# First batch's heads in three rounds of query tiles, with three token chunks behind them, and w1 loaded without a ring

## The reference

```python
scores = (1 / np.sqrt(D)) * np.matmul(q, k.transpose(0, 1, 3, 2))
cum = np.cumsum(np.maximum(s, 0.0), axis=-1)
bias = -(cum[:, :, :, None] - cum[:, :, None, :])
scores = np.where(causal, -1e9, scores + np.minimum(bias, 0.0))
attn = softmax(scores)                     # with 1e-9 added to the sum
x = np.matmul(attn, v)                     # then (2304 tokens, 512)
h = np.maximum(np.maximum(x @ w1, x @ w2), x @ w3)
y = h @ w_out                              # first layer, d_ff 768
out = ((y @ w_a) * (y @ w_b)) @ w_out2     # second layer, d_ff 1536
```

## Time and profile before

| | us |
|---|---|
| median of 3 runs | 985.52 (985.21 to 985.62) |
| the profiled execution | 985.47 |
| its span, first to last instruction | 983.7 |
| span covered by PE / PEld / DVE / ACT / POOL | 941.9 / 858.7 / 468.9 / 406.6 / 202.9 |

### The profile page before, as it was taken

The page is one execution under the profiler, slowest core; times in us unless marked ns, Lnnn a source line. Parts: engine busy times, 40 slices in busy tenths (PEclk is TensorE's granted clock), DMA queues, the critical chain, the costliest instruction groups (busy, mean ns, idle before and its releaser), DMA issues.

```text
span 983.7 us, 15197 instructions
## 1 busy us (share of the span) xinstructions
PE 941.9 (96%) x5776; PEld 858.7 (87%) x5776; DVE 468.9 (48%) x1054; ACT 406.6 (41%) x912; POOL 202.9 (21%) x293
## 2 busy tenths in 40 slices
PE   3688999999999999999999999999999999999998
PEld 2578899999999999999999888888888888888898
DVE  6689978877666577563323433221122112211222
ACT  4677777766655566543223333211121112111211
POOL 5556554444423324411000000000000000000000
PEclk9999999999999999999999999999999999999999
DMA  3544432222121221100032332100020001000100
GB/s 103 149 158 153 147 97 64 71 77 78 57 86 39 80 69 40 54 9 27 12 134 69 120 97 91 66 21 1 0 72 14 1 1 64 1 1 1 43 1 22
DMA packets 29240, 58.74 MB, mean 60 GB/s; under 512 B 3184, under 2 KB 15568, under 8 KB 29136
## 3 DMA queue, kind: packets, MB, share of 16 engines
q1 hardware_dynamic: 29168, 57.77, 18.6%
HBM read 47.87 MB, written 9.88 MB: 59 GB/s over the span
## 4 chain that ended last, share of the span: by engine, by line
PE 88%; DVE 5%; issue 4%; DMA 1%; POOL 1%; ACT 0%; SPq 0%; POOLq 0%; ACTq 0%; DVEq 0%
PE bank L1129 30%; PE bank L1008 21%; PE bank L1144 15%; PE bank L1027 8%; PE bank L960 5%; PE bank L990 5%; PE bank L976 4%; DVE soft L754 1%; DVE pt_lo L763 1%; DVE h_lo L794 1%; DVE qk_st L726 1%; DVE w_lo L732 1%; DMA cum_dram<-cum_row 0%; DVE qk_st L720 0%; DMA qk_raw<-in_qk 0%
## 5 line engine op out<-in xcount | busy, mean ns | idle before, releaser
L919 DVE TENSOR_TENSOR g_raw<-bank,a_sb 128x512 f32<-128x512 f32 (+1 forms) x60 | 38.3, 639 | 298.5 <-PE bank L1129 298.5
L1008 PE MATMUL bank<-xs_hi,w_hi 128*128 128x256 f32 (+1 forms) x576 | 173.9, 302 | 2.2 <-DVE xs_lo L775 1.5
L1008 PE MATMUL bank<-xs_hi,w_lo 128*128 128x256 f32 (+1 forms) x576 | 170.7, 296 | 0.0
L1008 PE MATMUL bank<-xs_lo,w_hi 128*128 128x256 f32 (+1 forms) x576 | 170.6, 296 | 0.0
L458 POOL TENSOR_SCALAR soft<-soft,rden 128x576 f32<-128x576 f32 (+4 forms) x160 | 102.7, 659 | 236.6 <-DVE rden L740 236.6
L1129 PE MATMUL bank<-y_hi,w2b_hi 128*128 128x512 f32 (+1 forms) x360 | 132.4, 368 | 0.0
L1129 PE MATMUL bank<-y_lo,w2b_hi 128*128 128x512 f32 (+1 forms) x360 | 132.4, 368 | 0.0
L1129 PE MATMUL bank<-y_hi,w2b_lo 128*128 128x512 f32 (+1 forms) x360 | 132.4, 368 | 0.0
L500 ACT ACTIVATE soft<-soft,neg_max 64x576 f32<-64x576 f32 (+4 forms) x160 | 96.1, 601 | 45.8 <-DVE neg_max L754 45.0
L1008 PEld LDWEIGHTS bank<-xs_hi,w_hi 128*128 128x128 f32 x576 | 109.3, 190 | 3.7 <-DVE xs_lo L775 1.7
L665 ACT ACTIVATE a_sb<-bank 128x512 f32<-128x512 f32 (+1 forms) x60 | 33.3, 555 | 188.5 <-PE bank L1129 188.5
(11 more groups left out here) (83 smaller groups left out, 1821.9 us busy)
## 6 DMA issues: line engine op xcount, KB each, us to landing
qk_raw<-in_qk SPq DMA_DIRECT2D x32, 576.0 KB, 3.8
w_raw<-in_w SPq DMA_DIRECT2D x40, 384.0 KB, 3.5
v_raw<-in_v SPq DMA_DIRECT2D x32, 160.0 KB, 2.2
y_raw<-y_dram SPq DMA_DIRECT2D x4, 1024.0 KB, 5.5
outT<-o_stage SPq DMA_DIRECT2D x16, 256.0 KB, 2.0
qk_raw<-in_qk SPq DMA_DIRECT2D x8, 256.0 KB, 3.1
y_dram<-m_tmp SPq DMA_DIRECT2D x8, 160.0 KB, 1.8
y_dram<-h_raw SPq DMA_DIRECT2D x8, 160.0 KB, 1.8
```

The source lines that it names most:

```text
L1008: ins = nc.tensor.matmul(up_ps[g][:, 0:width1(c)], up1_w(w, f, g, kc), x[:, kc, 0:width1(c)], start=(kc == 0 and at == 0), stop=(kc == KC ...
```

## The change

- Batch 0 is cut in three rounds in place of two: jobs 0 to 7 take tile 0, jobs 8 to 15 tile 1, jobs 16 to 23 tiles 2, 3, 4. Jobs 24 to 47 are the other batches.
- The chunks behind them are tokens 0 to 127, 128 to 255 and 256 to 575 of batch 0, then 256 and 320 tokens for each other batch, nine in all. The first three have eight slots each. The last chunk starts in slot 53 where it was slot 45.
- `w1_raw` becomes one whole buffer at the address of `w1_lo`, so loads wait for nothing. Pieces 0 to 6 are made in slots 1 to 7, the rest in slots 8 to 12. Of a piece DVE subtracts the first 512 columns and POOL the last 256 (`w1_rest_sub`), before it normalises the job of the slot.
- The bias rows of batch 0 come from the row in SBUF, and SP does not wait for `cum_dram` before job 2.
- In `alone_slot` ACT does `lower(n+1)` first, DVE `split_q` and `split_k` before `pt_lo_sub`.

```diff
+STAGES = [(0,), (1,), (2, 3, 4)]
+PARTIAL = HEADS * len(STAGES)
+N_JOBS = PARTIAL + N_HEADS - HEADS
 def tiles(n):
-    if n < HEADS:
-        return EARLY_TILES
-    return LATE_TILES if n < 2 * HEADS else tuple(range(QT))
+    return STAGES[n // HEADS] if n < PARTIAL else tuple(range(QT))
-CHUNK = [((0, SPLIT), (SPLIT, SEQ))[c % 2] for c in range(N_CH1)]
+CHUNK = [(0, P), (P, SPLIT), (SPLIT, SEQ)] + [(0, SPLIT), (SPLIT, SEQ)] * (BATCH - 1)
-FIRST = [9, 17, 25, 29, 33, 37, 41, 45]
+FIRST = [9, 17, 25, 33, 37, 41, 45, 49, 53]
-DENSE = 2
+DENSE = 3
-W1_PIECES = {2: [0], 4: [1], 8: [2, 3], 9: [4, 5], 10: [6, 7], 11: [8, 9], 12: [10, 11], 13: [12, 13], 14: [14, 15]}
+W1_PIECES = {n: [n - 1] for n in range(1, 8)}
+W1_PIECES.update({8: [7, 8], 9: [9, 10], 10: [11, 12], 11: [13, 14], 12: [15]})
+W1_SHARE = 512
...
+                w1_raw = early.enter_context(nc.sbuf_tensor("w1_raw", [P, W1_COLS], F32))
...
+            load_w1(0)
             sp.wait_ge(const_rows, 2)
             sp.wait_ge(cum_split, 1)
...
+            load_w1(1)
             sp.dma_start(cum_dram, cum_row[:, :, :].bitcast(F32)).then_inc(cum_stored, 16)
-            sp.wait_ge(cum_stored, 16)
...
-                if live(n + 2):
+                if n + 2 < HEADS:
+                    load_bias(n + 2, cum_row[n + 2:n + 3, :, :].bitcast(F32))
+                elif live(n + 2):
+                    if n + 2 == HEADS:
+                        sp.wait_ge(cum_stored, 16)
                     load_bias(n + 2, cum_dram[head(n + 2):head(n + 2) + 1])
-                for piece in W1_PIECES.get(n + 1, []):
-                    load_w1(piece)
+                for piece in W1_PIECES.get(n + 2, []):
+                    if piece > 1:
+                        load_w1(piece)
...
+            def w1_rest_sub(piece):
+                pool.wait_ge(w1_hi_done, piece + 1)
+                cols = slice(piece * PIECE + W1_SHARE, (piece + 1) * PIECE)
+                nc.gpsimd.tensor_tensor(w1_lo[:, cols], w1_raw[:, cols], w1_hi[:, cols].bitcast(F32), ALU.subtract
+                                        ).then_inc(w1_rest_done, 1)
...
                 if live(n):
                     split_v(n)
+                for piece in W1_PIECES.get(n, []):
+                    w1_rest_sub(piece)
                 if live(n):
                     for k in range(len(tiles(n))):
                         normalise(n, k)
```

## The result

| | us |
|---|---|
| before, median of 4 runs | 985.57 (985.21 to 985.63) |
| changed, median of 4 runs | 1047.51 (1045.66 to 1048.20) |
| ratio, 95% interval | 1.0626 (1.0608 to 1.0645) |
| changed, the profiled execution / its span | 1045.66 / 1043.9 |

The changed kernel is 62 us slower. I had forecast 24 slower, with 1037 as the upper end of my range. The direction was right and the size was not. Of the missing part 31 us are the rival that I had given 0.15: the first chunk stays at PE's low clock. That rival stood at 1039 us in my text; most of the rest lies in slots 0 to 8, which gained 10 us where I had 16.

The account below looks back on a forecast made before the run. A chain of short steps over all engines was taken to bound slots 0 to 8, and PE, nearly full, the later ones. Terms -16.1 + 46.4 - 6.1 = +24.2 us on 985.5 gave 1010 us, range 1001 to 1037.

Parts of the forecast that it names:

- the rival that I had given 0.15: Slots 9 to 16: PE stays at 1.2 GHz, 9.5 us a slot, +54 us, 1039 us in all; chance 0.15.
- slots 0 to 8: Start to job 7's output: first output at 13.4, then 3.3 us a slot; 16.1 us gained, bounds 8.4 and 18.9.
- three terms: Slots 0 to 8, -16.1 us; slots 9 to 16, +46.4; slots 17 to 24, -6.1; sum +24.2.
- Slots 9 to 16: Chunk 0 beside tile 1, new work for PE: 46.4 us added, bounds 41 and 55.
- the loop over w1: Slots 1 to 7: w1 copy, POOL's subtraction, multiplication, transpose and `pt_hi` form a loop of 2.95 us a slot.
- the loads as the second one: Slots 1 to 7: SP's loads form a second loop, 2.8 us a slot undelayed, a little more behind w1.
- My rival on the loads: Slots 1 to 8: w1 pieces queue ahead of q, k, v; 4.2 to 4.4 us a slot, 1017 to 1020; chance 0.12.
- Slots 17 to 24: Chunk 1 beside tiles 2, 3, 4: 73.8 us where the same jobs took 79.9; 6.1 gained, bounds 3 and 10.
- After that: From slot 25 on: the same order of work as before, so no term in the sum.
- The rule of the Trainium skill: Rival for 128-column matmuls: about 81 ns each, 17 us less, near 993 us; chance 0.03 for about 0.08 us.
- nearly doubles: Matmul price on PE: 0.11 us at 128 columns, 0.12 at 256, so two chunks of 128 cost nearly twice 256 tokens.
- The contention of DVE and POOL: Slots 1 to 7: simultaneous w1 subtractions might stretch 0.3 us each, loop 3.6 us, gain 14 us; not added.

## Why the prediction was wrong

The sum was made of three terms, so it can be checked at three points. "Clock up" is the run with 192 columns.

| job's output leaves PE at | predicted | clock up | changed |
|---|---|---|---|
| job 7 | 36.5 | 42.3 | 42.4 |
| job 15 | 82.9 | 88.7 | 119.8 |
| job 23 | 156.7 | 160.1 | 192.9 |
| whole kernel | 1010 | 1013.1 | 1047.5 |

- **Slots 9 to 16: the step that failed.** I let the low clock end in slot 9, as in the kernel before (5.15 + 4.1 us for it), and priced the seven slots behind it at the high clock: I had "44 at 0.11 are 4.9 us, and 5.15 with the longer steps" and a sum of 46.4 us. The stretch took 77.4, at a step of 0.213, 9.30 us a slot. With the clock up it is 46.4 us, the predicted value, and the slots without w1 take 4.9. So the sum held for a condition that was not met. That it holds to the tenth is in part luck: slot 12 makes one piece of w1 and not two as I wrote, slots 13 to 15 took 4.9 to 5.0 for my 5.15, and slot 16 took 6.0. The rival had it: 9.5 us a slot and 1039 us. I gave it 0.15 with the argument that PE "is hardly ever without" a matmul and "in the dense slots of before it never fell again". Neither says that narrow matmuls bring the clock up from below. The rise that I had seen came among 256-column matmuls and wider scores, and the level at the entry was the low one.
- **Slots 0 to 8.** I predicted 16.1 us gained, it was 10.2. The start is at 16.6 and not 13.4: ACT's copy for job 2 now stands ahead of its work on jobs 0 and 1 and waits 4.1 us for a load behind 800 KB (w1's second piece and `cum_dram`). The run with SP's new order confirms it: with those two behind the load, the first output came at 14.0. I had named the copy moved forward as a gain and not asked what it would wait for. Slots 1 to 7 took 3.7 us on average for my 3.3; I had the loop over w1 as the bound and the loads as the second one; by ACT's waits and the two runs on these slots it was rather the other way round. My rival on the loads (0.12) had named them, at 4.2 to 4.4 us a slot. The bounds, 8.4 and 18.9, held.
- **Slots 17 to 24.** Predicted 73.8, measured 71.4 with the clock up: 8.7 to 8.8 us a slot for my 9.1. In the changed kernel 73.1, since the clock rose within the first of them. With the clock up, slots 0 to 8 took 5.8 us more than predicted and this stretch 2.4 less; the two partly cancel in the whole.
- **After that**, no term: 851.0 for 851.2 us.
- **The rule of the Trainium skill** (TensorE: Matmul & The Clock Gate, Back-to-back issue gap) of about 81 ns a matmul for streams of 128 columns did not show in any run: with the clock up the step in streams of 128 columns was 0.11, apart from single steps of 0.06 to 0.08 where the line changes.
- **What I said of the price** ("nearly doubles") was true of PE's time and wrong as a cause: the extra loads lie beside a chain that needs 3.7 to 5.5 us a slot anyway. Leaving out the narrow chunk gave 2.6 us, so nearly all of the price came with the round, as far as a run tells in which those slots stood at the low clock.
- **The contention of DVE and POOL.** I added nothing for it; POOL's subtraction took 1.23 us beside DVE's and 0.73 without. The Trainium skill's statement (GPSIMD Engine Reference, Key points) agrees with this trace. No cost of it shows here: with the subtraction back at 0.72 us, job 7 left PE no earlier, though the multiplication then took part of the stretch.

## What to carry to other kernels

Before matmuls are made narrower, look at which clock level PE enters the stretch, and by the start times of matmuls, not by its busy share or the clock column. If it enters low, see that something wide stands there: padding 128 columns to 192 lengthened no step at either level and was worth 34 us here. When a round of work is cut in two to start the next layer earlier, count the new slots at the length of their dependency chain first; if the chain fills them, the work that they let in comes nearly free, and the slots themselves are the price.

## What the runs showed of the hardware that I had not expected

- PE ran 128-column float32r matmuls back to back for 77 us and never left 1.2 GHz; with 192 columns it was at 2.4 GHz after 7 us in slot 9. Once there, it stayed there over slots of 128 columns. In two runs it fell in the middle of slots 9 to 16: 2.3 us after PE had resumed from a wait of 1.70 us, and at a pause of 2.99 us.
- At both levels the weight load sets the step at 128 columns, 0.213 and 0.111 us, since 192 columns step the same. 256 columns step 0.213 and 0.120.
- The profile's clock column said 1.00 in the changed kernel for stretches at 1.2 GHz in which the level had not changed since the start, and 0.50 for the same level after a fall (81.5 to 97.3 us in the run with w1 in the old slots).
- A GpSimd subtraction of 256 columns took 1.23 us beside one on VectorE, and 0.72 to 0.73 without one; a multiplication of 128 columns there went from 0.37 to 0.82 us.
